# Gate and routing of the first expert stage taken in three batches, two of them inside the attention, with three early tiles for expert 0

## The reference

```python
attn_out = _attn_ref(q, k, v, mem_k, mem_v)        # B, H, S, D = 4, 8, 768, 64; chunks of 32, 16 left, 8 right, 8 memory rows
x = attn_out.transpose(0, 2, 1, 3).reshape(3072, 512)

logits = x @ w_gate                                  # first mixture
noisy = logits + log1p(exp(x @ w_noise)) * noise
top2 = argpartition(-noisy, 2)[:, :2]
w = exp(l - l.max()); w /= w.sum() + 1e-9            # l: the two chosen noisy logits
for e in range(8):                                   # each token with two experts
    out[mask] += w[mask, k, None] * (relu(x[mask] @ w1[e]) @ w2[e])

e = argmax(x2 @ w_gate2)                             # second mixture: one expert,
out[mask] = p[mask, e, None] * (relu(x2[mask] @ w1[e]) @ w2[e])   # weight: its softmax
```

## Time and profile before

| | us |
|---|---|
| median of 3 runs | 1260.9 (1256.64 to 1261.04) |
| the profiled execution | 1261.41 |
| its span, first to last instruction | 1259.6 |
| busy in it: PE / DVE / ACT / POOL | 1108.8 / 638.8 / 290.8 / 295.7 |
| mean granted PE clock | 0.924 |

### The profile page before, as it was taken

One profiled execution on the slowest core, in us unless ns is written; L12 is line 12 of the kernel. 1 busy time (PEld: TensorE's weight loads), 2 busy tenths in 40 slices (PEclk: granted clock), 3 DMA queues, 4 the chain that ended last, 5 costly groups with the idle time before them and its releaser, 6 DMA issues. The chain is left out here.

```text
span 1259.6 us, 29086 instructions
## 1 busy us (share of the span) xinstructions
PE 1108.8 (88%) x7956; PEld 911.8 (72%) x7957; DVE 638.8 (51%) x1189; ACT 290.8 (23%) x732; POOL 295.7 (23%) x380
## 2 busy tenths in 40 slices
PE   5888716899999999999999999947479999999995
PEld 4676615688888888888887888735367888887783
DVE  2455565555536354463555536405547535766850
ACT  4544422111212121212211212115202122112211
POOL 2000002132332233232332223210113222232221
PEclk9877756899999999999999999978589999999997
DMA  8877822576757566575667756528068646777951
GB/s 323 293 267 262 320 104 83 176 213 178 229 166 235 149 203 202 172 225 150 206 202 199 209 138 203 145 47 202 8 215 269 202 141 203 232 234 245 295 184 48
DMA packets 122113, 244.92 MB, mean 194 GB/s; under 512 B 14287, under 2 KB 67663, under 8 KB 122065
## 3 DMA queue, kind: packets, MB, share of 16 engines
q1 hardware_dynamic: 45360, 111.79, 26.8%
q10 hardware_dynamic: 58272, 83.96, 20.3%
q0 software_dynamic: 18432, 48.51, 15.8%
HBM read 168.97 MB, written 76.02 MB: 194 GB/s over the span
## 5 line engine op out<-in xcount | busy, mean ns | idle before, releaser
L1066 PE MATMUL moe_ps_y<-weights,moe_h_hi 128*128 x640 | 259.8, 406 | 13.8 <-DVE moe_h_lo L1196 13.2
L1066 PE MATMUL moe_ps_h<-weights,moe_x_hi 128*128 x640 | 254.6, 398 | 17.3 <-DVE moe_x_lo L1179 16.9
L1068 PE MATMUL moe_ps_h<-weights,moe_x_lo 128*128 x640 | 252.9, 395 | 0.0
L1067 PE MATMUL moe_ps_h<-weights,moe_x_hi 128*128 x640 | 252.5, 395 | 0.0
L1068 PE MATMUL moe_ps_y<-weights,moe_h_lo 128*128 x640 | 251.6, 393 | 0.0
L1067 PE MATMUL moe_ps_y<-weights,moe_h_hi 128*128 x640 | 251.6, 393 | 0.0
L1196 DVE SCALAR_TENSOR_TENSOR moe_h_lo<-moe_h_moved,moe_h_hi 128x256 fp32r<-128x256 f32 x320 | 114.4, 419 | 248.1 <-ACT moe_h_hi L1143 248.1
L1143 ACT ACTIVATE moe_h_hi<-moe_h_moved 128x1024 fp32r<-128x1024 f32 x80 | 84.9, 1062 | 392.1 <-PE moe_ps_y L1068 348.3
L418 DVE TENSOR_TENSOR weights<-stage,weights (+1 forms) x128 | 157.0, 1226 | 20.7 <-DVE weights L416 20.4
L1066 PEld LDWEIGHTS moe_ps_h<-weights,moe_x_hi 128*128 128x128 f32 x640 | 122.3, 191 | 48.3 <-issue 23.0
L1066 PEld LDWEIGHTS moe_ps_y<-weights,moe_h_hi 128*128 128x128 f32 x640 | 121.7, 190 | 38.8 <-issue 15.7
(11 more groups left out here) (158 smaller groups left out, 869.8 us busy)
## 6 DMA issues: line engine op xcount, KB each, us to landing
stage<-in_w SPq DMA_DIRECT2D x128, 512.0 KB, 3.4
h_d<-moe_h_turned ACTq DMA_DIRECT2D x80, 512.0 KB, 2.9
moe_h_moved<-h_d ACTq DMA_DIRECT2D x320, 128.0 KB, 3.0
k_sb<-in_k SPq DMA_DIRECT2D x24, 512.0 KB, 6.7
v_sb<-in_v SPq DMA_DIRECT2D x24, 512.0 KB, 4.9
x_d<-zero SPq DMA_DIRECT2D x26, 256.0 KB, 4.2
q_sb<-in_q SPq DMA_DIRECT2D x24, 256.0 KB, 5.5
x_d<-x_sb POOLq DMA_DIRECT2D x24, 256.0 KB, 5.7
```

The costliest lines, as they stand in the source:

```text
L1066: pe.matmul(out, a_hi, b_hi, start=(i == 0), stop=False)
L1067: pe.matmul(out, a_hi, b_lo, start=False, stop=False)
L1068: mm = pe.matmul(out, a_lo, b_hi, start=False, stop=(i == len(parts) - 1))
```

## The change

The blocks `attention`, `choose_one`, first `route` and first `experts` become one block, `front`. The noisy choice and the routing of the first mixture are done in three batches of 8 tiles: batch 0 in attention tiles 9 to 14, batch 1 in tiles 17 to 22, batch 2 among the first expert tiles. A pair's place is now its expert and its rank in that expert; per place one matmul sum gives the row of x to take, so `routes.row` has 8 x 24 columns of places, and the tables `place` and `expert` say which column a tile uses and which gate column. Gate weights no longer go through the route's matmuls: each batch writes its 8 weights per token behind the token's 512 values in `x_d` (rows of 520), the gather brings them, and POOL's `keep_gate` copies the right one out. The first three tiles of expert 0 are taken from batches 0 and 1 alone (`early`); if there were fewer than 384 such pairs, `late` would leave holes. Pads move to the front of `x_d` and `x2_d`. Weight pieces are split in tiles 4 to 8, 15, 16 and 23; the rate for the later ones is 3 per tile. The second mixture keeps its blocks; its loop code is the same.

```diff
+NB = 3
+BT = 8
+EARLY = 3
+PLACES = E * NT
+    STARTS = [b * BT + BT + 1 for b in range(2)]
+    EXP = {t + 1: b for b, t in enumerate(STARTS)}
+    LN = {t + 2: b for b, t in enumerate(STARTS)}
+    PROB = {t + 3: b for b, t in enumerate(STARTS)}
+    RANK = {t + 3: b for b, t in enumerate(STARTS)}
+    PLACE = {t + 5: b for b, t in enumerate(STARTS)}
+    PIECE_IN = {6: 4, 8: 5, 10: 6, 12: 7}
+    PIECE = {4: 0, 5: 1, 6: 2, 7: 3, 8: 4, 15: 5, 16: 6, 23: 7}
...
+            for t in range(NT - 1):
+                store_x(t)
+                if t - 5 in STARTS:
+                    store_gates(STARTS.index(t - 5))
+            for i in range(NB):
+                pool.wait_ge(sem(f"x_out{i}"), 16 * ((2 * BT - 1 - i) // NB + 1))
+            pool.wait_ge(sem("gates_out"), 32)
+            pool.wait_ge(sem("x_pad"), 16)
+            pool.wait_ge(sem("early_rows"), 1)
+            x.gather(pool, 0)
+            store_x(NT - 1)
+            for t in range(1, EARLY):
+                pool.wait_ge(s("xt_done"), t)
+                x.keep_gate(pool, t - 1)
+                x.gather(pool, t)
+            store_gates(2)
...
+            pool.wait_ge(sem("x2_zero"), 16 * (NT + 2))
+            x.scatter(pool, 0)
+            pool.wait_ge(sem("gates_out"), 48)
+            pool.wait_ge(sem("routed"), 1)
+            m = x.tiles(pool)
+            for t in (EARLY, EARLY + 1):
+                pool.wait_ge(s("xt_done"), t)
+                x.keep_gate(pool, t - 1)
+                x.gather(pool, t)
+            x.pool_loop(pool, 1, m)
...
+            def places(b):
...
+                for i in range(2 * BT):
+                    if i % BT == 0:
+                        pe.wait_ge(sem("hot_ready"), 2 * b + i // BT + 1)
+                    for a in range(2):
+                        mm = pe.matmul(bt.ps_sum, bt.hot_r[:, i, a, :], bt.hot_p[:, i, :], start=(i == 0 and a == 0),
+                                       stop=(i == 2 * BT - 1 and a == 1))
...
+                values(t)
+                if t in RANK:
+                    pe.wait_ge(sem("const_route"), 1)
+                    ranks(RANK[t])
+                if t in PLACE:
+                    places(PLACE[t])
+            x_transposes(NT - 1)
+            gate(NT - 2).then_inc(sem("s_done"), 1)
+            x.x_transposes(pe, 0)
+            gate(NT - 1).then_inc(sem("s_done"), 1)
+
+            pe.sem_inc(s("turned"), 2)
+            x.first_product(pe, 0)
+            x.x_transposes(pe, 1)
+            x.first_product(pe, 1, between=lambda: ranks(2))
+            x.x_transposes(pe, 2)
+            x.first_product(pe, 2)
+            x.second_product(pe, 0)
+            places(2)
+            x.second_product(pe, 1)
+            pe.wait_ge(sem("routed"), 1)
+            m = x.tiles(pe)
+            x.x_transposes(pe, 3)
+            x.first_product(pe, 3)
+            x.x_transposes(pe, 4)
+            x.tensor_loop(pe, 3, m)
...
+            x.high_x(act, 0)
+            noise_exp(2)
+            noise_ln(2)
+            x.high_x(act, 1)
+            x.park(act, 0)
+            gate_exp(2)
+            x.high_x(act, 2)
+            x.fetch(act, 0)
+            x.park(act, 1)
+            x.high_h(act, 0)
+            x.fetch(act, 1)
+            x.park(act, 2)
+            x.high_h(act, 1)
+            x.weigh(act, 0)
...
+            def hots(b, kk):
...
+                for t in range(BT):
+                    i, token = kk * BT + t, b * BT + t
+                    slot = bt.slot[:, kk, t:t + 1]
+                    dve.tensor_scalar(bt.hot_p[:, i, :], c["iota_b"][:, :], bt.place[:, kk, t:t + 1], None,
+                                      ALU.is_equal)
+                    dve.tensor_scalar(bt.hot_r[:, i, 0, :], c["iota_b"][:, 0:P], slot, c["token"][:, 0:1],
+                                      ALU.is_equal, ALU.mult)
+                    ins = dve.tensor_scalar(bt.hot_r[:, i, 1, :], c["iota_b"][:, 0:P], slot, float(P * (token + 1)),
+                                            ALU.is_equal, ALU.mult)
...
+                if t in PIECE:
+                    weight_piece(PIECE[t])
+                for b, start in enumerate(STARTS):
+                    if t == start:
+                        dve.wait_ge(sem("const_route"), 1)
+                        noise_size(b)
+                    if t == start + 1:
+                        noise_plus(b)
+                    if t == start + 2:
+                        noise_scale(b)
+                        choose_two(b)
+                    if t == start + 3:
+                        rank_slots(b)
+                        hots(b, 0)
+                    if t == start + 4:
+                        hots(b, 1)
+                        gate_weights(b)
+                    if t == start + 5:
+                        add_places(b)
+                        if b == 1:
+                            rows(routes.early[:, :], EARLY).then_inc(sem("early_rows"), 1)
+            copy_xT(NT - 1)
+            for t in (NT - 2, NT - 1):
+                copy_logits(t)
...
+            noise_size(2)
+            x.low_x(dve, 0)
+            noise_plus(2)
+            noise_scale(2)
+            choose_two(2)
+            x.turn(dve, 0)
+            x.low_x(dve, 1)
+            rank_slots(2)
+            x.turn(dve, 1)
+            x.low_x(dve, 2)
+            hots(2, 0)
+            x.low_h(dve, 0)
+            hots(2, 1)
+            x.turn(dve, 2)
+            gate_weights(2)
+            expert_tables(dve, c, tt, step, total, bt, routes, tables)
+            x.low_h(dve, 1)
+            add_places(2)
+            rows(routes.row[:, :], PLACES).then_inc(sem("routed"), 1)
...
+    def keep_gate(self, pool, t):
+
+        if isinstance(t, int) and t < EARLY:
+            at = self.xg[:, DM:DM + 1]
+        else:
+            at = self.xg[:, bass.ds(self.table(pool, self.routes.expert, t, DM, DM + E - 1), 1)]
+        pool.tensor_copy(self.routes.gate[:, bass.ds(t, 1)], at).then_inc(self.s("gated"), 1)
+
+        pool.wait_ge(self.s("gated"), t + 1)
...
+            pool.wait_ge(s("xt_done"), t + 4)
+            pool.nop(nofuse=True)
+            if self.routes.early is not None:
+                self.keep_gate(pool, t + 3)
+            self.gather(pool, t + 4)
+            self.scatter(pool, t)
```

More of the change, by code:

```diff
@@ L407, in load_piece @@
+    step(pool.tensor_scalar(c["source_row"][:, :], c["token"][:, 0:1], float(N + P), None, ALU.add))
+    pool.sem_inc(sem("const_route"), 1)
 def load_piece(eng, sem, stage, w, e, j):
@@ new lines, in add_places, with rows @@
+            def add_places(b):
+                dve.wait_ge(sem("place_done"), b + 1)
+                if b == 0:
+                    ins = dve.tensor_copy(bt.sum[:, :], bt.ps_sum)
+                else:
+                    ins = dve.tensor_tensor(bt.sum[:, :], bt.ps_sum, bt.sum[:, :], ALU.add)
+                ins.then_inc(sem("place_read"), 1)
+                dve.wait_ge(sem("place_read"), b + 1)
+            def rows(out, n):
+                step(dve.tensor_scalar(bt.empty[:, 0:n], bt.sum[:, 0:n], 0.0, c["token"][:, 0:1],
+                                       ALU.is_equal, ALU.mult))
+                return dve.tensor_tensor(out, bt.sum[:, 0:n], bt.empty[:, 0:n], ALU.add)
@@ L1271, in moe_of_attention @@
[L1271 to L1276 removed]
+            with scratch_ctx:
+                att = Attention(nc, sem, scratch)
+                bt = Batches(scratch, att.ps_x, gates)
+                tables = Tables(scratch, routes[0].cols)
+                end = scratch("scratch_end", [P, 8])
```

1347 lines of the change are left out of this document (795 added, 552 removed).

## The result

The changed kernel takes 1316.0 us (median; 1311.3 to 1318.9), the kernel before beside it 1259.4: ratio 1.0448, 95% interval 1.0409 to 1.0488. The forecast was 1247.5 with a range to 1264: wrong in sign and size, by 68.5 us. The profiled execution took 1318.9 (span 1317.2, clock 0.911).

What follows compares the result with a forecast made beforehand. TensorE work bounds the expert stages, so only the 56.0 us gap before the first expert product could be won. 1261.4 - 32.5 + 19.0 = 1247.9, stated as 1247.5; range 1231 to 1264.

Steps and rivals of the forecast that it cites:

- Part 1: Tail between the last attention output and the first expert product: all 56.0 us leave the path, replacements costed separately.
- Part 2: Attention tiles: the batched choice, ranking and places work adds 14 us, bounds 5 and 24; last output near 173.4.
- some 4 us: Attention: how much later the sum would be if ACT table loads also cost the skill's drain of about 1.4 us.
- Part 3: From last attention output to first expert product: 9.5 us, bounds 6 and 15; product at 183, 32.5 earlier than before.
- Part 4: First expert tiles: late fetch, batch-2 routing work and PE waits lose 19.0 us, bounds 12 and 26.
- Part 5: Expert loop: more weight pieces per tile cost nothing, and POOL's added 1.3 to 1.9 us per tile fit its slack.
- PE waits for gathers in the loop at all: Sign that the forecast is wrong: any TensorE wait for gathered rows in the expert loop.
- Rate 3 ... has cover ...: nothing.: Expert loop: 3 weight pieces per tile instead of 2 add up to 2 us to a DVE tile, at no cost.
- It fits, barely.: POOL's expert loop: added steps of 1.3 to 1.9 us per tile against slack of 1.65.
- rival D: POOL's serial loop bounds the first expert stage; 0.5 over in 48 tiles gives +19, so 1266.5 us; chance 0.11.

## Why the prediction was wrong, point by point

**Part 1, the tail: right.** It went whole; nothing of it is in the new timeline.

**Part 2, the attention: right, a little low.** +16.7 against 14, bounds 5 to 24. The lumps are where they were put: outputs of tiles 11 to 14 are 8.6, 8.7 and 7.8 us apart. Against the kernel before, the outputs of tile 11 are 1.0 us late, those of tile 19 7.6, and those of tile 23 16.7: 6.6 for batch 0 (6.1 was forecast), 9.1 for batch 1 (8.5), and 1.0 ahead of both, which was put at nothing. The cost that was short is `hots`. One slot after (DVE, timeline):

```profile
160.59 0.26 DVE L918 TENSOR_SCALAR hot_p<-iota_b,rank_place 128x192 bf16<-128x192 bf16 x1
160.76 0.31 DVE L920 TENSOR_SCALAR hot_r<-iota_b,rank_slot,token 128x128 bf16<-128x128 bf16 x1
160.99 0.25 DVE L922 TENSOR_SCALAR hot_r<-iota_b,rank_slot 128x128 bf16<-128x128 bf16 x1
...
172.47 0.36 DVE L944 TENSOR_TENSOR places<-ps_x,places 128x192 f32<-128x192 f32 x1 [3.97 <-PE ps_x L642]
```

Their starts are 0.17, 0.23 and 0.16 apart, so a call of 24 takes 4.5 us, not 3.0: at 0.19 each bf16 halved nothing against the 0.20 of the earlier trace rows. `places` is seen with 3.97, where I took 3. `hots` made each batch 3.0 short, and yet its three stretched tiles took 25.1 and 25.4 us against the forecast's 24.6: the choice (6.5), `rank_slots` (2.0), the gate weights (1.25) and the tiles' own DVE work (2.2, not 2.77) took less, and there errors cancel. The table loads are costed right at nothing: in tile 11 they stand at 83.58 and 85.15, 1.28 each, while DVE is in its choice until 91.70. Those of batch 2:

```profile
185.07 1.28 ACT L717 ACT_TABLE_LOAD   x1
186.37 0.26 ACT L717 ACTIVATE noisy<-noisy 128x64 f32<-128x64 f32 x1
```

The Ln starts 0.02 after the load's end here too; the drain that the Trainium skill adds (ScalarE: Activation LUTs, What ACT_TABLE_LOAD costs) isn't seen in the changed kernel either. (My "some 4 us" was no clean sum of it: four loads in the attention at 1.4 each would be 5.6, an estimate from that page.)

**Part 3: right.** The first product starts 9.36 us after the last output's end; 9.5 was forecast. The transposes that wait for the gather start 5.6 after that end, a little later than the 4 to 5 costed for its landing.

**Part 4: right in sum, off in its parts.** PE waits 6.96 before the second of the early second-products, where 4 was forecast (the second one), and 0.25 before the first. From the first product to tile 5 the lead shrinks from 29.9 to 12.8, by 17.1 against 19.0. So the lead is 12.8 against the forecast's 13.5, with two errors of opposite sign in it: the attention took 2.7 more, and these tiles 1.9 less.

**Part 5, the loop: wrong, and it is the whole error.** Its term in the sum was nothing; 69.2 us were measured. Of the signs of being wrong, "PE waits for gathers in the loop at all" is the one that came true. Three steps failed.
- "Rate 3 ... has cover ...: nothing." It was argued from DVE's time and from the second stage. But the second stage has neither gate copy nor register loads in POOL's ring. The rate's cost isn't a wait for DVE: in the changed kernel's loop PE never waits for it. With the longer ring the cost is there in the changed kernel (48.3: 56.6 at 3 splits, 8.3 at 2) and as much in the kernel before with POOL's steps (47.7: 72.3 and 24.6); without those steps it is 4.6.
- "It fits, barely." The slack of 1.65 and added steps of 1.3 to 1.9 leave 0.3 at best; 0.46 is measured, or 0.20 had the tiles kept their 11.37. The register load was priced from PE's queue; POOL's has the same 0.29 in the median, but is over 0.5 for 32 of 144. An average slack says nothing of tiles in which several long DVE instructions fall on POOL's copies; there the ring is 1.45 over. The stretching could have been read in the trace of before, where gathers of 1.08 reach 1.48 and copies of 0.18 reach 0.67 beside splits.
- In rival D a microsecond over cost a microsecond. In the tile shown 1.45 over cost 3.8, as the clock falls behind the wait. Over the stage, 29 of the 48 periods are longer than 11.7, by 2.00 over 11.63 on average.

So rival D had the place and, with the stretching and the clock left out, the mechanism, and 0.11 of the chance, with 19 us where 69 was measured. The term that was mis-sized is its 48 tiles x 0.5: measured 48 x 1.44, of which 1.20 over the tiles' 11.63. The slower pitch, which no rival had, adds nothing while the ring is late. With both taken away, parts 1 to 4 stand: the version with the landing wait moved and the rows padded runs in 1244.0, 3.5 from the forecast. That it is so near is partly luck: the errors above cancel, and this version reaches tile 5 2.7 us earlier than the changed kernel (249.56).

The Trainium skill (SBUF — State Buffer, SBUF: two separate sides) says that a DVE instruction with two SBUF inputs and a GpSimd instruction that reads SBUF take a shared port pair in turn, each for its whole length. This case agrees: the POOL copy that starts at 529.03 lasts 1.23 beside the DVE subtraction of two SBUF tiles at 529.00 with 1.22, and 0.18 where it is alone. In the changed kernel from 260 to 820 us all 26 copies that begin during such a subtraction end 0.04 to 0.05 us behind its end, after 0.35 to 1.22 us. DVE being busy isn't enough: beside instructions that read PSUM the copies keep their length. So it is in all 77 cases of the version with the landing wait moved, as in these rows:

```profile
600.52 1.30 DVE L1574 STREAM_TRANSPOSE moe_h_turned<-moe_ps_h 128x512 f32<-128x512 f32 x2
600.88 0.18 POOL L1432 COPY routes_gate<-moe_xg  x1 [2.60 <-PE moe_ps_x L1462]
601.75 0.65 DVE L1563 TENSOR_TENSOR moe_x_lo<-moe_ps_x,moe_x_hi 128x512 fp32r<-128x512 f32 x1
601.85 0.19 POOL L1416 COPY moe_from_row<-routes_row 128x1 int32 x1 [0.79 <-POOL routes_gate L1432]
```

In the kernel before, a split's first instruction, with one SBUF input, held 28 copies in the same way (up to 0.65), which that sentence doesn't name. So the traces show that these DVE instructions, whose operands all lie in SBUF, hold POOL's copies to their end; the port as the reason is the page's. No run here changed the splits' form and kept their number, so how much of the 69 us this holding makes is argued; that splits and POOL's steps together make the loss is shown.

## What to carry to other kernels

- A queue that closes a ring (issue, landing, copy, issue) is costed as a ring against the period, and in its worst tile, not by its mean wait: ask what long instruction of another engine can fall on each of its steps, and what the change does to how these bunch.
- Wait for a transfer where its buffer is needed again, not where it was issued: that alone was worth 59 us here.
- Don't take "a higher rate runs in the other stage" as cover: ask whether the queues there have the same steps.
- When a row gets wider, look at what is allocated behind it. Here padding it was worth 12.7 us, but only once the ring was mended.

## What the runs showed of the hardware that I had not expected

- A matmul of 512 columns with fp32r operands has a pitch of 0.2267 to 0.2288 us where the stationary operands lie 0, 256 or 512 bytes over a multiple of 1024 behind the start of the moving ones, and 0.2330 to 0.2334 where they lie 32 over (0.2321 to 0.2335 at 128 over): 2.6% on average. Why is open.
- A POOL copy of 128x1 takes 0.18 us alone and up to 1.27 beside a DVE weight split, to whose end it is held; beside DVE instructions that read PSUM it stays at 0.18 to 0.19. The issue of an indirect gather goes from 1.08 to 2.09.
- A scatter with addition lands 5.5 us after the start of its issue in the median (4.7 to 6.3, all 53 of the changed kernel), of which the issue itself is 1.61.
- A register load on POOL takes 0.29 us in the median, and up to 1.61.
- A wait of PE of 1.13 us cost 3.8, with a granted clock of 0.88 in the 14.2 us behind it.
- bf16 one-hots of 128 and 192 columns cost 0.16 to 0.23 us each, 0.19 on average, about as much as f32 ones of 128 with 0.20.
